# Attention, token mixer and channel mixer on one core: both rounds' down products by seven quarter products

## The reference, cut to what matters

```python
x  = attention(q, k, v)                      # 4 batches x 448 tokens x 768 features
u  = x + token mixing of x; u = u + relu(u @ w_ch)
xt = u.transpose(0, 2, 1)
h  = np.maximum(xt @ w_tok1, 0.0) @ w_tok2   # 448 -> 256 -> 448, over the tokens
u  = u + h.transpose(0, 2, 1)
h2 = np.maximum(u @ w_ch1, 0.0) @ w_ch2      # 768 -> 1536 -> 768, over the features
out = u + h2
```

## Time and profile before

| | |
|---|---|
| median of 3 runs | 823.44 us |
| the profiled execution | 822.83 us, span of its instructions 821.0 us |
| PE busy | 813.9 us, 99% |
| DVE, ACT, POOL busy | 618.6, 427.0, 149.6 us |
| granted clock of PE | full in every slice |
| channel stage, round 0's rise, its fall, round 1's rise, its fall begin at | 356, about 515, 579.5, 665.8, 741.5 us |

### The profile page before, as it was taken

The page is one execution under the profiler, slowest core; times in us unless marked ns, Lnnn a source line. Parts: engine busy times, 40 slices in busy tenths (PEclk is TensorE's granted clock), DMA queues, the critical chain, the costliest instruction groups (busy, mean ns, idle before and its releaser), DMA issues.

```text
span 821.0 us, 12996 instructions
## 1 busy us (share of the span) xinstructions
PE 813.9 (99%) x4906; PEld 702.7 (86%) x4906; DVE 618.6 (75%) x971; ACT 427.0 (52%) x622; POOL 149.6 (18%) x132
## 2 busy tenths in 40 slices
PE   8999999999999999999999999999999999999998
PEld 6555555589999999999999999999999999999997
DVE  5899999989977675865657579777512767779885
ACT  6999999947565554812213134444211624457551
POOL 0355556332000000024333000000563000000000
PEclk9999999999999999999999999999999999999999
DMA  7556764344321221326673643533687545443443
GB/s 181 162 142 165 192 168 132 92 110 120 97 68 49 59 68 39 116 87 185 224 215 122 184 125 110 183 112 111 201 270 232 192 151 175 147 142 107 145 122 128
DMA packets 106541, 115.55 MB, mean 141 GB/s; under 512 B 38672, under 2 KB 104176, under 8 KB 106480
## 3 DMA queue, kind: packets, MB, share of 16 engines
q1 hardware_dynamic: 106256, 114.50, 47.6%
q10 hardware_dynamic: 224, 0.23, 0.1%
HBM read 85.73 MB, written 28.96 MB: 140 GB/s over the span
## 4 chain that ended last, share of the span: by engine, by line
PE 89%; DVE 6%; issue 2%; ACT 2%; POOL 0%; DVEq 0%; POOLq 0%; ACTq 0%
PE psum L1684 25%; PE psum L1686 25%; PE psum L1685 25%; PE psum L1740 6%; PE psum L1696 4%; PE psum L1767 2%; PE psum L1698 1%; DVE tile_sums L1165 1%; ACT ring L910 1%; ACT ring L913 1%; PE psum L1775 1%; DVE kq_lo L1152 1%; DVE u_lo L1325 0%; DVE kq_hi L1150 0%; DVE sum_rows L1187 0%
## 5 line engine op out<-in xcount | busy, mean ns | idle before, releaser
L1360 DVE TENSOR_TENSOR part_lo<-part_raw,part_hi 128x384 fp32r<-128x384 f32 x150 | 85.5, 573 | 45.7 <-ACT part_hi L1007 45.7
L1007 ACT ACTIVATE part_hi<-part_raw 128x384 fp32r<-128x384 f32 x150 | 74.1, 516 | 81.1 <-DMA part_raw<-moe_w_ch 53.7
L1684 PE MATMUL psum<-block_hi,part_hi 128*128 128x448 f32 x252 | 91.5, 363 | 0.0
L1686 PE MATMUL psum<-block_hi,part_lo 128*128 128x448 f32 x252 | 91.3, 362 | 0.0
L1685 PE MATMUL psum<-block_lo,part_hi 128*128 128x448 f32 x252 | 90.8, 360 | 0.0
L1740 PE MATMUL psum<-ring,values 128*32 128x448 f32 x768 | 81.5, 542 | 0.6 <-issue 0.5
L910 ACT ACTIVATE ring<-psum,score_scale 128x1344 f32<-128x1344 f32 (+1 forms) x48 | 75.3, 1569 | 8.1 <-PE psum L1698 4.8
L913 ACT ACTIVATE ring<-ring,cap_col 128x1344 f32<-128x1344 f32 (+1 forms) x48 | 77.2, 1607 | 1.6
L1740 PEld LDWEIGHTS psum<-ring,values 128*32 128x32 f32 x768 | 23.4, 109 | 42.7 <-issue 42.7
L1684 PE MATMUL psum<-theta_hi,x_hi 128*128 128x384 f32 x168 | 56.4, 335 | 0.0
L1686 PE MATMUL psum<-theta_hi,x_lo 128*128 128x384 f32 x168 | 56.1, 334 | 0.0
(11 more groups left out here) (190 smaller groups left out, 2223.4 us busy)
## 6 DMA issues: line engine op xcount, KB each, us to landing
part_raw<-moe_w_ch SPq DMA_DIRECT2D x78, 192.0 KB, 2.3
kq_raw<-kq_t SPq DMA_DIRECT2D x47, 224.0 KB, 3.8
part_raw<-quad_scratch SPq DMA_DIRECT2D x48, 192.0 KB, 2.4
values<-v SPq DMA_DIRECT2D x48, 112.0 KB, 3.4
inverse_rows<-inverse_scratch SPq DMA_DIRECT2D x12, 448.0 KB, 6.4
rows_scratch<-turned SPq DMA_DIRECT2D x112, 48.0 KB, 1.7
x_rows<-rows_scratch SPq DMA_DIRECT2D x28, 192.0 KB, 2.3
block_scratch<-block_turned SPq DMA_DIRECT2D x32, 168.0 KB, 3.5
```

The lines of the kernel that those rows point to most:

```text
L1007: act.activation(part_hi[SLOTS[q]][:, :], part_raw[SLOTS[q]][:, :], ACT.Copy).then_inc(part_hi_made, 1)
L1360: dve.tensor_tensor(part_lo[slot][:, :], part_raw[slot][:, :], part_hi[slot][:, :].bitcast(F32), ALU.subtract).then_inc(part_lo_made, 1)
L1684: pe.matmul(out, left[0], right[0], start=start, stop=False)
L1686: return pe.matmul(out, left[1], right[0], start=False, stop=stop)
```

## The change

Round 0's fall takes the seven products of round 1's, 42 parts and 378 matmuls in place of 24 and 432. Its rise therefore keeps `h_raw` and makes sums (`sum_rises`) instead of low parts (`relu_to_lo`). The weight sums for the falls are needed earlier: POOL makes them in the channel stage, one whole quad `fall_quads` behind each rise quad, in the place where the raw token weights lay, so that the first load waits for `tok_split`. The operands of round 0's seven products lie where round 1's blocks go; so these blocks are loaded into places that become free in the fall, summed there, and the last one, B22, is rounded at the start of round 1's rise.

```diff
@@ SyncE
+            def load_fall_quads(pair):
+                if pair == 0:
+                    sp.wait_ge(tok_split, 2)
+                after(sp, fall_quads_stored, 16 * pair)
+                sp.dma_start(fall_quads[:, :, :], w_ch2[pair].rearrange("m k p n -> p (m k) n")
+                             ).then_inc(fall_quads_loaded, 16)
+            def store_fall_quads(pair):
+                sp.wait_ge(fall_quad_steps, 4 * (pair + 1))
+                sp.dma_start(fall_quad_scratch[pair].rearrange("q p n -> p q n"), fall_quads[:, :, :]
+                             ).then_inc(fall_quads_stored, 16)
...
             load_quads(0)
+            load_fall_quads(0)
             for j in range(HALVES - 1):
                 store_squares(j)
                 load_block_rows(j)
...
                     store_quads(j)
                 if j + 1 < C_PAIRS:
                     load_quads(j + 1)
+                if j < C_PAIRS:
+                    store_fall_quads(j)
+                if j + 1 < C_PAIRS:
+                    load_fall_quads(j + 1)
...
@@ GpSimd
+            for pair in range(C_PAIRS):
+                sum_quads(pair, quads, quads_loaded, quad_steps)
+                sum_quads(pair, fall_quads, fall_quads_loaded, fall_quad_steps)
...
@@ ScalarE
+            def last_block_to_hi():
+                act.wait_ge(part_read, fall_part(0, M3, D_PAIRS - 1, 1) + 1)
+                for k in range(K_PAIRS):
+                    rounded = act.activation(block_hi[B22][:, k, :], b22_raw[k][:, :], ACT.Copy)
+                rounded.then_inc(block_hi_made, 1)
...
@@ VectorE
+            def fall(s):
+                for g in range(4, C_PAIRS):
+                    seven_to_lo(s, M1, g)
+                for m in M_ORDER:
+                    for step in range(2 * D_PAIRS):
+                        part_to_lo(fall_part(s, m, 0, 0) + step + 3)
+                        if m == M1 and 1 <= step < 5:
+                            sum_rises(s, C_PAIRS - 1, (M7, M6, M4, M5)[step - 1])
+                        if m != M3:
+                            seven_to_lo(s, M_ORDER[M_ORDER.index(m) + 1], step)
+                        if step % 2 == 1:
+                            add_fallen(s, m, step // 2)
+                        if s == 0 and m == M4 and step in (1, 3):
+                            sum_next_blocks((T3, T2)[step // 2])
+                        elif s == 0 and m == M5 and step == 5:
+                            block_to_lo(1, B11)
+                        elif s == 0 and m == M3 and step == 1:
+                            sum_next_blocks(T4)
+                            block_to_lo(1, B21)
+                        elif s == 0 and m == M3 and step == 2:
+                            sum_next_blocks(T1)
+                        elif s == 0 and m == M3 and step == 3:
+                            block_to_lo(1, T2)
+                        elif s == 0 and m == M3 and step == 5:
+                            block_to_lo(1, T3)
...
@@ TensorE
-                if s == 0:
-                    for p in range(2):
-                        for g_half in range(2):
-                            for k in range(2):
-                                for e in range(3):
-                                    fall(p, g_half, k, e)
-            for m in M_ORDER:
-                for pair in range(D_PAIRS):
-                    fall_by_seven(m, pair)
+                for m in M_ORDER:
+                    for pair in range(D_PAIRS):
+                        fall(s, m, pair)
```

More of the change, by code:

```diff
@@ L320, in h_tile @@
             return 4 * g + 2 * m_half + n_half
-        fall_quads = [place(f"fall_quads{e}", [P, 4, HALF // 2], F32, block_at[T2 + e]) for e in range(QUAD_BUFFERS)]
+        fall_quads = place("fall_quads", [P, 4, HALF], F32, AT_TOP + 52224 + PHASE)
+        b12_raw = [place(f"b12_raw{k}", [P, SEQ], F32, h_at[h_tile(k, 0, 0)] + 1792) for k in range(K_PAIRS)]
+        b11_raw = [place(f"b11_raw{k}", [P, SEQ], F32, h_at[h_tile(k, 1, 0)] + 1792) for k in range(K_PAIRS)]
+        b22_raw = [place(f"b22_raw{k}", [P, SEQ], F32, h_at[h_tile(*tile)] + 1792)
+                   for k, tile in enumerate(((3, 0, 0), (4, 0, 0), (5, 1, 0)))]
         seven_at = {M1: [h_at[h_tile(g, 0, 0)] + 1792 for g in range(C_PAIRS - 1)]
@@ L434, in mixer_kernel @@
         quads_stored = sem("quads_stored")
-        blocks_loaded = sem("blocks_loaded")
+        blocks_loaded = [sem(f"blocks_loaded{e}") for e in range(2)]
         block_sums_made = sem("block_sums_made")
@@ new lines, in load_block_tile, with load_first_blocks @@
+            def load_block_tile(group, raw, d, n):
+                sp.dma_start(raw[:, :], spilled_rows[:, d, n * SEQ:(n + 1) * SEQ]).then_inc(blocks_loaded[group], 16)
+            def load_first_blocks():
+                sp.wait_ge(spilled, 32)
+                sp.wait_ge(part_read, fall_part(0, M1, D_PAIRS - 1, 1) + 1)
+                for k in range(K_PAIRS):
+                    load_block_tile(0, b12_raw[k], 2 * k, 1)
+                for k in range(2):
+                    load_block_tile(0, b22_raw[k], 2 * k + 1, 1)
+                load_block(B11, block_raw[B11], 0)
@@ L756, in reload_x, with load_second_blocks @@
+            def load_second_blocks():
+                sp.wait_ge(part_read, fall_part(0, M2, D_PAIRS - 1, 1) + 1)
+                load_block_tile(1, b22_raw[2], 5, 1)
+                for k in range(K_PAIRS):
+                    load_block_tile(1, b11_raw[k], 2 * k, 0)
+                load_block(B21, block_raw[B21], 0)
             def reload_x(piece):
@@ L890, in _, with sum_quads @@
-            for h in range(HALF_QUADS):
-                sum_half_quads(h)
+            def sum_quads(pair, buffer, loaded, steps):
+                pool.wait_ge(loaded, 16 * (pair + 1))
+                a11, a12, a21, a22 = [buffer[:, e, :] for e in range(4)]
+                pool.tensor_tensor(a22, a21, a22, ALU.add).then_inc(steps, 1)
+                pool.wait_ge(steps, 4 * pair + 1)
+                pool.tensor_tensor(a21, a11, a21, ALU.subtract).then_inc(steps, 1)
+                pool.wait_ge(steps, 4 * pair + 2)
+                pool.tensor_tensor(a11, a22, a11, ALU.subtract).then_inc(steps, 1)
+                pool.wait_ge(steps, 4 * pair + 3)
+                pool.tensor_tensor(a12, a12, a11, ALU.subtract).then_inc(steps, 1)
@@ L1944, in fall_by_seven, with fall @@
[L1944 removed]
+            def fall(s, m, pair):
                 r = D_PAIRS * M_ORDER.index(m) + pair
[L1947 to L1948 removed]
+                if r < 2 and s == 0:
+                    pe.wait_ge(u2_made, D_TILES * BATCH)
+                elif r < 2:
+                    pe.wait_ge(fall_adds_made, fallen(0, M3, r + 1))
                 elif r < 8:
[L1950 removed]
+                    wait_until_read(s, C_PAIRS - 1, M_ORDER[r - 1])
```

429 lines of the change are left out of this document (159 added, 270 removed).

## The result

The changed kernel takes **841.43 us** (median of 4 runs, 840.12 to 842.3), the kernel before, on the same chip, 823.23 (4 runs, 822.66 to 824.46): ratio 1.0218, interval 1.02 to 1.0236. The forecast was 834.7, with a range up to 840. The direction and the place are as forecast, the size is not: the loss is half as large again. The profiled execution took 840.12 us, with a span of 838.1.

What follows compares the result with a forecast made beforehand. The prediction took the number of matmuls PE issues as the bound, with any new PE stall adding in full. 822.83 - 10.8 + 1.1 + 21.6 = 834.7 us, range 824.5 to 840.

Steps and rivals of the forecast that it cites:

- Fewer matmuls: First round's fall: 432 matmuls become 378, 54 x 0.200 us saved, -10.8 us.
- First round's rise, ACT, POOL at nothing: Sums replacing low parts in the rise, ACT's roundings, and POOL's extra channel-stage sums: each claimed to add zero.
- Turn of the rounds: Start of the second round's rise: DVE finishes B22's low parts after PE wants them, +1.1 us, bounds 0 and 4.
- SyncE's queue: Channel stage: added transfers and landing waits delay squares and rows, so PE stops; +21.6 us accumulated.
- X: Landing time of the new fall_quads store in SyncE's list: taken as 6.0 us, ends 4.4 and 6.6.
- the upper row: Trace row of squares stored behind a just-issued load, landing after 7.0 us against 4.4; source of the 6.6 end.
- the 5.33 of the earlier trace: DVE's time for six low parts of half 4's u tiles, within the 7.46 us from tiles to down-token products.
- Around the span: Start of the sum: profiled 822.83 us, span 821.0 plus 1.8; the median's 0.6 above the profiled time left out.
- More cover: Rival, channel stage: SyncE's queue has more cover than seen, change is faster, 812 to 813 us; chance 0.10.
- Transfers that don't hinder each other: Rival, channel stage: queue costs only +12.5 us, 825 to 827 us with block wait; chance 0.15.
- The clock: Rival: PE's clock falls to 1.2 GHz in the last stop, 2 to 5 us more, 837 to 840; chance 0.17.
- DVE late at the turn: Rival, turn of the rounds: block lumps stall PE 4 us or more instead of 1.1, 838 to 840; chance 0.06.

Runs made afterwards that it cites:

- experiment 2: Kernel before plus only the fall's whole-quad transfers and POOL sums in the channel stage, both falls unchanged: 850.21 us, ratio 1.0323.
- experiment 4: Changed kernel with POOL's sums of the fall's quads cut to 2 of 384 columns, all transfers kept: 842.35 us, ratio 1.023.
- experiment 8: Against experiment 5, DVE makes B22's low parts before the addition and weight part ahead of them: 828.22 us, ratio 1.006.
- experiment 3: Changed kernel with ACT rounding the hidden tiles ahead of the next half's rows: 841.77 us, ratio 1.0226.
- experiment 9: Changed kernel with the fall quads' loads and stores issued by POOL behind its sums, SyncE's list as before: 823.47 us, ratio 0.9993.
- experiment 6: Changed kernel with SyncE's order altered: behind squares and rows come the last half's two quad stores, then this half's loads: 821.88 us, ratio 0.9977.
- experiment 12: Against experiment 10, the last pair's quad loads go behind half 6's rows, its stores behind the rise's first weight parts: 818.49 us, ratio 0.9926.
- experiment 1: Changed kernel with SyncE storing both quads behind the next half's squares and loading the next quads behind the rows: 830.9 us, ratio 1.0091.
- 5: Changed kernel with SyncE's order altered: both quad loads ahead of the rows, both stores behind them: 828.62 us, ratio 1.006.
- 7: Changed kernel with 91 extra matmuls, results unread, meant to fill PE's three channel-stage stops: 840.42 us, ratio 1.0206.
- 11: Against experiment 10, quad loads of pairs 1 to 5 issued by POOL once the store before has landed: 825.16 us, ratio 1.001.
- experiment 10: Against experiment 6, DVE makes B22's low parts one place earlier: 820.11 us, ratio 0.9955.

## Why the prediction was right and where it missed

The measured time is 1.4 us above the upper end of the range. The step that failed is the size of the term for SyncE's queue, with the clock beside it.

- *Fewer matmuls, -10.8 us.* Right: 378 matmuls in 76.0 us, and experiment 2 against the changed kernel gives 8.8 with 1.9 of new gaps.
- *First round's rise, ACT, POOL at nothing.* Right for the time. PE has no new wait in the rises but at the turn, and POOL's sums of the fall's quads cut to two columns change nothing (experiment 4).
- *Turn of the rounds, +1.1.* Right: 1.36, and 0.7 of it went away with B22's low parts earlier (experiment 8). The gap early in each fall costs 0.5 us, and the first fall's is new; I had nothing for it.
- *SyncE's queue, +21.6.* This is the mis-sized term: 25.8. Mechanism and place were right, the stops only in part: forecast 9.8, 2.2, 2.2 and 7.7 us, measured 10.3, 2.3, none and 6.9. The third is missing because slow matmuls had made PE late by then. The four squares' stores were forecast 1.3, 1.5, 2.4 and 4.3 us too early. Two assumptions carried that. X was taken as 6.0, "a little better spaced" than the upper row; it is 6.6 to 6.8, at or above the upper end. The ring order that the Trainium skill (DMA: Bandwidth & Descriptors, "Queues, rings and completion order") states had pointed to that end. Over four halves that is 2.8 us. And the quad store was held at its 4.4 us of before, though in the new list it also lands beside more traffic: 5.8, 4.7, 5.0, 6.3 us, 4.2 more in all. The first half's rows, 0.9 earlier than forecast, and shorter steps around them take back the rest: the squares of half 4 leave 4.3 us too late. Behind them two errors cancel: the low parts took 2.0 us less than the 5.33 of the earlier trace rows, and the slow matmuls, which the sum had at nothing, gave 2.0 back. I had bounded the new transfer from both sides and left the old ones at their old price; so the upper end, 840, was 1.4 us too low.
- *Around the span.* The profiled execution is 2.0 us above its span and the median 1.3 above that; I had added 1.8 and nothing. 4.2 of the queue, 0.8 of the two gaps, some 0.4 of rounding and surroundings, and 1.3 between median and profile make up the 6.7 us.
- *The rivals.* More cover: no, experiment 3 shows that cover only moves the stops. Transfers that don't hinder each other: no, by every landing above. The clock: in part. It falls to 0.50 behind all three stops, and it adds some 2 us behind the last, the low end of the 2 to 5 that I gave it; 841.4 less 2 would lie inside the range. In experiment 9 it costs 2.6. The length of a stop alone doesn't tell whether it falls: behind the 2.3 us of the changed kernel and the 2.1 of experiment 6 it did, behind the 3.1 of experiment 12 it didn't. DVE late at the turn: no.

The best version still has some 5 us more than the sum without stops: its span is 816.5 us, where 821.0 - 10.8 and the 1.2 of its two gaps make 811.4. The stop at 490 is 3.3 of them. The down-token products of halves 0 to 4 start 0.5 to 0.9 us later than before. And in the first fall DVE, level with PE in my count, is the bound for a moment, as these two windows of experiment 12 show (10 us each; 52 matmuls are PE's pace):

```profile
625.71:635.71 10.00, 10.00 (x52) 9.37 (x51) 9.93 (x20) 5.95 (x13) 0.00 (x0) 1.00 0.36 103
635.71:645.71 10.00, 9.82 (x48) 8.30 (x47) 10.00 (x19) 8.67 (x13) 0.00 (x0) 1.00 0.51 163
```

DVE has no idle time there and PE starts in steps of 0.3 to 0.5 us. In the changed kernel the same place keeps its 52 matmuls in both windows. The list of this fall is the same in all experiments from the changed kernel on, but at this place experiments 1, 5, 6, 7 and 9 have 46 to 48 in the second window, 11 has 50, and 8 and 10 have 52. So the list alone doesn't tip it; what does, no experiment tried.

## What to carry to other kernels

A queue that issues in order and waits for landings has a period: add up the landings between two uses of the same step and compare the sum with the consumer's period, before looking at bytes or bandwidth. If it is longer, change the order first: stores that are issued together land side by side, where a wait between them adds their landings up, and here the same transfers cost 19.6 us less so (experiment 6). When transfers are added to such a list, price the old ones anew as well, and keep the one that PE waits for free of large loads just ahead of it or just behind, from whichever queue.

## What the runs showed of the hardware

**DVE and POOL slow each other.** Six low parts of 128 x 448 take DVE 5.33 us before, where POOL sums a quad at the same time, 3.30 in the changed kernel, where POOL is idle, and 7.38 in experiment 1, where POOL sums all along; its own operations, 1.02 us elsewhere, are then 1.3:

```profile
470.57 3.30 DVE L1305 TENSOR_TENSOR u_lo<-x_t,u_hi 128x448 fp32r<-128x448 f32 x6 [9.24 <-ACT u_hi L953]
```

```profile
453.66 7.38 DVE L1303 TENSOR_TENSOR u_lo<-x_t,u_hi 128x448 fp32r<-128x448 f32 x6 [1.94 <-ACT u_hi L951]
```

```profile
455.24 1.27 POOL L854 TENSOR_TENSOR quads<-quads 128x384 f32<-128x384 f32 x1
456.59 1.27 POOL L856 TENSOR_TENSOR quads<-quads 128x384 f32<-128x384 f32 x1
```

DVE needs 1.23 us for an operation of 0.55, and POOL starts one every 1.35. The Trainium skill (SBUF — State Buffer, "SBUF: two separate sides") says that the two engines hold a shared pair of ports by turns, whole instructions long, when DVE has two inputs in SBUF and POOL's operation reads it. The trace agrees that each waits for the other, six operations of one beside six of the other. But 0.55 and 1.02 make 1.57 us, more than the 1.35 of a pair, so not quite the whole lengths exclude each other. So the row on which the 7.46 us of the forecast rested held 2 us of POOL's work.

**A landing depends on its neighbours.** The four squares' stores, 32 x 14 x 96 each, let the rows go after 4.4 to 4.7 us with nothing large beside them, after 7 us behind one quad's load, 7.6 to 9.4 behind two (experiments 6, 10 and 12; the longest in experiment 10, 466.09 to 475.50), and 12.7 with a store just ahead and two loads issued behind them from the other queue.
